# Head 0's attention operands made in place, with q and k loaded a second time with halves exchanged

## What is computed

```python
q_bits = (np.einsum('bhsd,dk->bhsk', q, proj) > 0)      # 6 bits; k_bits in the same way
mask = q_bucket[:, :, :, None] == k_bucket[:, :, None, :]
scores = np.where(mask, scale * q @ k.T, -1e9)
attn = softmax(scores); out = attn @ v
```

## Time and profile before

| | us |
|---|---|
| median of the runs | 743.95 |
| the profiled execution, its device time | 744.51 |
| its span from the first to the last instruction | 742.7 |
| PE busy in the span | 716.0 |
| DVE busy | 427.9 |
| ACT busy | 336.6 |
| POOL busy | 322.8 |

### The profile page before, as it was taken

The page is one execution under the profiler, slowest core; times in us unless marked ns, Lnnn a source line. Parts: engine busy times, 40 slices in busy tenths (PEclk is TensorE's granted clock), DMA queues, the critical chain, the costliest instruction groups (busy, mean ns, idle before and its releaser), DMA issues.

```text
span 742.7 us, 10815 instructions
## 1 busy us (share of the span) xinstructions
PE 716.0 (96%) x3754; PEld 604.6 (81%) x3754; DVE 427.9 (58%) x731; ACT 336.6 (45%) x689; POOL 322.8 (43%) x284
## 2 busy tenths in 40 slices
PE   3999999999998999999999999999999999999998
PEld 2788888888887877788888888888888888888876
DVE  2899999999999777733122121211333556845443
ACT  1899989988987834433210111121223344123101
POOL 3688878878887339855100000020033564221100
PEclk9999999999999999999999999999999999999999
DMA  6464753444332012423000000110011210000002
GB/s 162 117 146 113 176 146 84 99 113 100 88 73 66 1 44 64 135 85 100 0 1 1 0 1 2 41 57 22 1 42 44 85 50 29 1 28 15 15 28 86
DMA packets 39399, 45.76 MB, mean 62 GB/s; under 512 B 15796, under 2 KB 26676, under 8 KB 39348
## 3 DMA queue, kind: packets, MB, share of 16 engines
q1 hardware_dynamic: 36564, 41.65, 20.5%
q0 software_dynamic: 2784, 3.43, 1.8%
HBM read 28.16 MB, written 3.15 MB: 42 GB/s over the span
## 4 chain that ended last, share of the span: by engine, by line
PE 76%; DVE 15%; issue 4%; ACT 2%; DMA 1%; POOL 1%; SPq 0%; ACTq 0%; POOLq 0%; DVEq 0%
PE PS L890 21%; PE PS L892 21%; PE PS L891 21%; DVE negmax L1237 6%; DVE ETL L1247 4%; DVE affine L1240 3%; PE PS L1021 2%; PE PS L981 2%; PE PS L1007 2%; PE PS L1006 2%; PE PS L1022 2%; PE PS L1109 1%; ACT OS L787 1%; PE PS L1036 1%; PE PS L992 1%
## 5 line engine op out<-in xcount | busy, mean ns | idle before, releaser
L1390 DVE SCALAR_TENSOR_TENSOR HL<-PS,HH 128x512 fp32r<-128x512 f32 x48 | 33.1, 691 | 154.7 <-ACT HH L876 154.7
L775 ACT ACTIVATE E<-PS,affine 128x768 f32<-128x768 f32 x96 | 95.2, 992 | 38.8 <-DVE affine L1240 36.1
L876 ACT ACTIVATE HH<-PS 128x512 fp32r<-128x512 f32 x48 | 28.7, 598 | 180.9 <-PE PS L892 180.9
L1237 DVE TENSOR_REDUCE negmax<-PS 128x1 f32<-128x768 f32 x96 | 90.8, 946 | 16.9 <-PE PS L1007 15.8
L1247 DVE TENSOR_TENSOR ETL<-PS,ETH 128x384 fp32r<-128x384 f32 x192 | 97.0, 545 | 2.5 <-ACT ETH L768 2.5
L981 PE MATMUL PS<-ident,E 128*128 128x128 f32 x576 | 81.8, 275 | 2.2 <-DVE ETL L1247 2.1
L768 ACT ACTIVATE ETH<-PS 128x384 fp32r<-128x384 f32 x192 | 82.7, 486 | 0.9 <-PE PS L981 0.8
L1021 PE MATMUL PS<-ETH,VHL 128*128 128x384 f32 x192 | 72.3, 377 | 5.2 <-ACT OS L787 4.7
L890 PE MATMUL PS<-UTH,W 128*128 128x512 f32 x192 | 75.8, 395 | 0.2 <-issue 0.2
L1006 PE MATMUL PS<-TOPH,TOPL 128*128 128x512 f32 x192 | 69.1, 360 | 6.5 <-DMA KM<-MR 6.2
L892 PE MATMUL PS<-UTH,W 128*128 128x512 f32 x192 | 74.8, 390 | 0.0
(11 more groups left out here) (173 smaller groups left out, 1572.2 us busy)
## 6 DMA issues: line engine op xcount, KB each, us to landing
RAW<-in_moe_w_ch_dram SPq DMA_DIRECT2D x32, 256.0 KB, 2.7
QK<-in_qk_dram SPq DMA_DIRECT2D x16, 384.0 KB, 3.8
QM<-TOPH SPq DMA_DIRECT2D x16, 192.0 KB, 2.9
KM<-TOPL SPq DMA_DIRECT2D x16, 192.0 KB, 3.2
VR<-in_v_dram SPq DMA_DIRECT2D x16, 192.0 KB, 2.7
TOPL<-QM SPq DMA_DIRECT2D x16, 192.0 KB, 2.7
TOPH<-TOPH SPq DMA_DIRECT2D x16, 192.0 KB, 3.0
out_dram<-fin SPq DMA_DIRECT2D x12, 256.0 KB, 2.0
```

The source lines that it names most:

```text
L775: nc.scalar.activation(E[:, tile % NE, :], s_bank(tile)[:, 0:S], ACT.Exp, bias=affine[:, t, 1:2], scale=affine[:, t, 0:1], accum_out=esum[ ...
L1237: nc.vector.tensor_reduce(negmax[:, t, 1:2], s_bank(tile)[:, 0:S], AX_X, ALU.max, negate=True).then_inc(s_max, 1)
```

## The change

Head 0 no longer passes through the move DMAs and the mask DMAs.

- The host lays q and k of head 0 into the input a second time, k above q. The load goes to a slice of `E` that is first written by tile 2's exponentials (`turned`). From `QK` and `turned` each of the eight pieces is then made on the partitions where it is used: ACT writes `QM[0:64]` and `TOPL[64:128]`, DVE `TOPL[0:64]`, POOL both halves of `TOPH` and `KM[0:64]`.
- The bits of head 0 come from two matmuls on the fp32 `QK` with the fp32 `proj2`, into a score bank. `proj2` has 44 columns in place of 24: the 12 of q, 20 of zeros, and the 12 of k from column 32 on.
- DVE compares them from PSUM straight into `QM[64:76]` and `KM[64:76]`.
- Two matmuls over a block of zeros stand first on PE.
- ACT's queue issues the three constants; DVE's product of `proj2` waits for two of them.
- Head 1 is split by ACT and DVE in the way of head 0 before, not by POOL. `MB`, `MR` and all bits products have 44 rows in place of 24, for every head.

```diff
@@ sync
             load_qk(0)
-            sp.dma_start(proj2[:], projb).then_inc(s_const, 16)
-            sp.dma_start(sign[:], sign_in).then_inc(s_const, 16)
-            sp.dma_start(gamma[:], gamma_in).then_inc(s_const, 16)
+            sp.dma_start(E[:, NE - 1, :], qk[NH]).then_inc(s_turned, 16)
             load_qk(1)
+            load_v(0)
             sp.dma_start(ident[:], ident_in).then_inc(s_ident, 16)
-            move_away(0)
-            load_v(0)
-            move_in(0)
-            move_mask(0)
             load_qk(2)
             load_v(1)
@@ gpsimd
+            pool.memset(E[:, 0, 0:HC], 0.0).then_inc(s_blank, 1)
...
-            scale_q(1)
+            turned = E[:, NE - 1, :]
...
+            pool.wait_ge(s_qk[0], 16)
+            nc.gpsimd.tensor_copy(TOPH[D:P, 0], QK[D:P, 0]).then_inc(s_first_key, 1)
+            pool.wait_ge(s_turned, 16)
+            nc.gpsimd.tensor_copy(TOPH[0:D, 0], turned[0:D]).then_inc(s_first_key, 1)
+            pool.wait_ge(s_first_key, 2)
+            nc.gpsimd.tensor_tensor(KM[0:D, 0], turned[0:D], TOPH[0:D, 0].bitcast(F32), ALU.subtract).then_inc(s_first_key, 1)
+            pool.wait_ge(s_first_key, 3)
+            split_v(0)
@@ scalar
+            act.dma_start(proj2[:], projb).then_inc(s_const, 16)
+            act.dma_start(sign[:], sign_in).then_inc(s_const, 16)
+            act.dma_start(gamma[:], gamma_in).then_inc(s_gamma, 16)
             act.wait_ge(s_qk[0], 16)
+            nc.scalar.activation(QM[0:D, 0], QK[0:D, 0], ACT.Copy, scale=SCALE).then_inc(s_first_high, 1)
+            act.wait_ge(s_turned, 16)
+            nc.scalar.activation(TOPL[D:P, 0], E[D:P, NE - 1, :], ACT.Copy, scale=SCALE).then_inc(s_first_high, 1)
+            act.wait_ge(s_qk[1], 16)
             act.wait_ge(s_init, 2)
-            nc.scalar.activation(TOPH[:, 0], QK[:, 0], ACT.Copy, scale=qscale[:]).then_inc(s_top, 1)
+            nc.scalar.activation(TOPH[:, 1], QK[:, 1], ACT.Copy, scale=qscale[:]).then_inc(s_top, 1)
@@ tensor
+            blank = E[:, 0, 0:HC]
+            pe.wait_ge(s_blank, 1)
+            for _ in range(2):
+                nc.tensor.matmul(OT, blank[:, 0:P], blank, start=True, stop=True)
+            pe.wait_ge(s_proj, 1)
+            pe.wait_ge(s_qk[0], 16)
+            nc.tensor.matmul(s_bank(1)[0:MW, 0:512], proj2[:], QK[:, 0, 0:512], start=True, stop=True)
+            nc.tensor.matmul(s_bank(1)[0:MW, 512:S], proj2[:], QK[:, 0, 512:S], start=True, stop=True).then_inc(s_first_bits, 1)
...
+                    if tile == 0:
+                        pe.wait_ge(s_first_high, 2)
+                        pe.wait_ge(s_first_key, 3)
+                        pe.wait_ge(s_first_low, 1)
+                        pe.wait_ge(s_first_mask, 2)
@@ vector
-            dve.wait_ge(s_const, 16 * 3)
+            dve.wait_ge(s_const, 16 * 2)
             nc.vector.tensor_tensor(proj2[:], proj2[:], sign[:], ALU.mult).then_inc(s_proj, 1)
...
+            dve.wait_ge(s_first_high, 1)
+            nc.vector.scalar_tensor_tensor(out=TOPL[0:D, 0], in0=QK[0:D, 0], scalar=SCALE, in1=QM[0:D, 0].bitcast(F32),
+                                           op0=ALU.mult, op1=ALU.subtract).then_inc(s_first_low, 1)
+            dve.wait_ge(s_gamma, 16)
+            dve.wait_ge(s_first_bits, 1)
+            nc.vector.tensor_scalar(QM[D:D + NM, 0], s_bank(1)[0:NM, 0:S], gamma[0:NM, 0:1], gamma[0:NM, 1:2], ALU.is_gt,
+                                    ALU.mult).then_inc(s_first_mask, 1)
+            nc.vector.tensor_scalar(KM[D:D + NM, 0], s_bank(1)[KROW:MW, 0:S], gamma[KROW:MW, 0:1], gamma[KROW:MW, 1:2], ALU.is_gt,
+                                    ALU.mult).then_inc(s_first_mask, 1)
```

More of the change, by code:

```diff
@@ L24 @@
 NM = 2 * BITS
+KROW = 32
+MW = KROW + NM
 SCALE = D ** -0.5
@@ L61, in schedule @@
 def schedule():
-    slots = [(None, None, None, [("bits", 0, i) for i in range(2)])]
+    slots = [(None, None, None, [])]
     for n in range(NH * QT):
@@ L108, in program @@
     einv = put("einv", [P, NSTAT])
[L109 to L113, removed]
+    sign = put("sign", [P, MW])
+    proj2 = put("proj2", [P, MW])
+    projH = put("projH", [P, MW], F32R)
+    projL = put("projL", [P, MW], F32R)
+    gamma = put("gamma", [MW, 2])
     stats = put("stats", [P, NT, 6])
@@ L127, in program @@
     region = used[0]
-    MB = put("MB", [2 * NM, S], F32, un_at)
+    MB = put("MB", [MW, S], F32, un_at)
     src_at = tail - 4 * 2 * DM
@@ L158, in program @@
     KM = put("KM", [D + NM, 2, S], F32R)
-    MR = put("MR", [2 * NM, S], F32R)
+    MR = put("MR", [MW, S], F32R)
     VR = put("VR", [P, 2, QT, D])
@@ L550, in split_top @@
                 b, r = h % 2, h % 3
-                pool.wait_ge(s_sq, h)
-                pool.wait_ge(s_top, 2 * h)
+                pool.wait_ge(s_sq, h - 1)
+                pool.wait_ge(s_top, 2 * (h - 1))
                 if h >= 3:
@@ L794, in _ @@
                             act.wait_ge(s_mr, h - 1)
-                        nc.scalar.activation(MB[:, c], ring(unit_no[u])[0:2 * NM, 0:HC], ACT.Copy).then_inc(emptied["bits"], 1)
+                        nc.scalar.activation(MB[:, c], ring(unit_no[u])[0:MW, 0:HC], ACT.Copy).then_inc(emptied["bits"], 1)
                     elif kind == "back":
@@ L984, in unit @@
                     c = slice(i * HC, (i + 1) * HC)
-                    pe.wait_ge(s_top, 2 * (h + 1))
-                    if h == 0 and i == 0:
+                    pe.wait_ge(s_top, 2 * h)
+                    if h == 1 and i == 0:
                         pe.wait_ge(s_proj, 3)
-                    last = product(bank[0:2 * NM, 0:HC], projH[:], TOPH[:, h % 3, c], projL[:], TOPL[:, h % 3, c], True, True)
+                    last = product(bank[0:MW, 0:HC], projH[:], TOPH[:, h % 3, c], projL[:], TOPL[:, h % 3, c], True, True)
                 elif kind == "back":
@@ L1255, in _ @@
                     kind, h, i = u
[L1256 to L1261 removed]
+                    if kind == "s1" and i < 2:
                         half_low(0, i)
@@ L1431, in constants @@
         "ident": np.eye(P, dtype=np.float32),
-        "gamma": np.array([[0, 1]] * BITS + [[-TINY, 1]] * BITS + [[-TINY, -PEN]] * BITS + [[0, -PEN]] * BITS, dtype=np.float32),
-        "sign": np.tile(np.repeat(np.array([[1, -1, -1, 1]], dtype=np.float32), BITS, axis=1), (P, 1)),
+        "gamma": np.array([[0, 1]] * BITS + [[-TINY, 1]] * BITS + [[0, 0]] * (KROW - NM) + [[-TINY, -PEN]] * BITS + [[0, -PEN]] * BITS, dtype=np.float32),
+        "sign": np.tile(np.concatenate([np.repeat([1, -1], BITS), np.zeros(KROW - NM), np.repeat([-1, 1], BITS)]).astype(np.float32), (P, 1)),
         "cs": parts(wave(np.cos, np.arange(S // 2), np.arange(KC), S)),
```

64 lines of the change are left out of this document (35 added, 29 removed).

## The result

The changed kernel takes 742.45 us (median of 17 runs, 741.87 to 743.09), the kernel before beside it 743.93 (17 runs, 743.7 to 744.83). The ratio is 0.998 with a 95% interval of 0.9973 to 0.9988: faster by 1.5 us, where 8 were forecast, and outside the range. The profiled execution took 742.71, its span is 740.4; PE is busy for 720.3 us of it, DVE 433.2, ACT 338.2, POOL 322.4.

What follows compares the result with a forecast made beforehand. Bound by the chain of waits, mostly DMA round trips, before the first score matmul at 14.73 us. An earlier start (6.2) plus clock (1.9) made 8.1 off, forecast 736.0 us, range 734.2 to 740.5.

Steps and rivals of the forecast that it cites:

- T0: Start of the first score matmul: forecast at 8.5 us in place of 14.73, 6.2 earlier, bounds 7.7 to 10.4.
- the clock: PE in the early slots: rises to 2.4 GHz before the first scores and stays, 1.9 us gained, ends 0 and 2.3.
- What bounds the kernel: Start to first scores: mostly three DMA round trips in a row; starting earlier ends the kernel earlier by as much.
- Constants: Loads issued by ACT: second lands at 3.95, with DVE's product 4.2; bounds 3.8 and 5.1 us.
- Order on DVE: DVE before the first scores: head 0's low part runs 4.75 to 5.75, under the bits' matmuls.
- Bits: Head 0's fp32 products on PE: 2.1 us, 4.2 to 6.3; bounds 0.8 and 3.1, or 2.8 by four passes.
- Masks: DVE's two comparisons from PSUM for head 0: 1.07 us each, 6.35 to 8.4, no DMA following.
- cold start: Rival, PE at first scores: still or again at 1.2 GHz, only 6.2 gained, 737.8 us; chance 0.28.
- Reload: Rival, POOL before its subtraction: code library reload of over 1 us delays first scores, middle 739.5 us; chance 0.12.
- POOL paying for rows: Rival, POOL's comparison on 44 rows: grows 2.4 us a head, some 10 us lost, 746; chance 0.04.
- No effect: Rival, after the start: a later wait at an absolute time swallows the gain, 743 to 744 us; chance 0.04.

Runs made afterwards that it cites:

- the delay: Changed kernel with head 0's comparison of q made four times, each waiting for the one before: 745.84 us, ratio 1.0024 to the kernel before.
- the run with wider rows: Kernel before with only the masks' rows widened to 44: 744.79 us, ratio 1.0014 to the kernel before.
- the version of 739.14: Changed kernel with ACT making the signs, projH/projL behind the comparisons, POOL's KM subtraction behind DVE's low part, two more matmuls over zeros between bits and scores: 739.14 us.
- that of 740.51: The version of 739.14 with proj2 on MB's place and no sign tile, so large buffers keep the addresses of the kernel before: 740.51 us, ratio 0.9943.
- the run over zeros: Changed kernel with four matmuls over zeros ahead of the bits and two behind them: 741.90 us, ratio 0.9972 to the kernel before.

## Why the prediction was wrong, point by point

In one line: T0 came 3.35 later than the sum had it, the clock gave nothing of 1.9, and 0.55 was lost behind; 8.1 less these is 2.3, the difference of the two profiled spans (742.7 and 740.4).

**What bounds the kernel: right.** T0 sets the end, and shifts pass nearly one to one (3.53 in, 3.4 out by the delay; 2.85 left at tile 6, 2.62 at tile 95). What it missed is 0.25 us in the heads and 0.3 behind them. The second goes with the addresses; of the first the rows have the larger part, as far as one profile of each version tells, and by a way that stays open. I had costed the rows at nothing and had not thought of addresses.

**Constants: wrong by 1.5 us.** The signs landed at 5.45, not 3.95. Issued at 1.17, as I said, they took 4.28, not `gamma`'s 2.73. My upper bound (5.1) was too low. I chose the row of a load that had gone out behind one big load, where now it leaves on another queue while two big loads are under way. The loads of head 0's q and k and of head 1's took 4.1 in place of 3.3 in the same stretch, and the first constant 3.6. The size of the load is not the reason, by the run with wider rows. Which of the two, the queue or the company, costs the time was not taken apart. It was the first link of the path, so all of it counted.

**Order on DVE: the step that failed by its mechanism.** "4.75 to 5.75, under the bits" for the low part could not be: in program order it stands behind the wait for the signs and three instructions on `proj2`. It came at 8.56. I had costed the product at 0.25 us and the other two at nothing, and POOL held each of them to its own end. The product cost 0.55 more before the bits, and the queue made the comparisons start at 9.54, 0.5 behind the bits in place of 0.05. The rule on the shared port was to be read in the Trainium skill (SBUF — State Buffer, Who interferes with whom), and the case was visible: the change puts POOL's subtraction and DVE's small work at the same time for the first time.

**Bits: a size, 0.7 us.** 2.79 from first start to end, where I took 2.1. The 1.73 between the starts is four times 0.43, as by the rule of the Trainium skill that I cited (FP8 and Floating Point Precision, TensorE Precision Notes; "T0 would be 0.7 later"). It lay inside my bounds; I weighed a row of another operation above the only source on this one. The two matmuls over zeros were dear in the same way, 1.46 each (1.49 to 4.42) and not 0.3, but the bits started only at 6.25.

**Masks: right**, 1.07 each, with 1.10 between their starts and 0.15 to the first matmul, 0.15 more than I had. The sum of the misses: 1.5 + 0.55 + 0.7 + 0.45 + 0.15 = 3.35, and 8.5 became 11.86.

**The clock: nothing of 1.9, the largest single miss.** The step that failed is "PE is busy from 1.5 to 6.3 nearly without a break" and then only about 2 us idle. PE stood still for 1.83 before the bits, which ran at the lower clock, and for 2.81 before T0. Even where the clock was up at the bits, it was down at the scores after 2.63. The rival "cold start" had the outcome; its 0.43 between the first scores is what the trace shows. It had T0 at 8.5 too, so its 737.8 was still 4.7 off. Where the scores did run at the higher clock, the lasting worth was about 0.9, half of my term: tile 4 came 7.87 behind T0 where my chain had 6.9, and tile 6 12.54 where it had 11.3.

**The other rivals: dead.** Reload: POOL's subtraction starts 0.08 us behind the cast (6.14 to 6.22), with the reload between them in program order. The 6 us of the Trainium skill (GPSIMD Engine Reference, Instruction dispatch) are not seen here. POOL paying for rows: 2.93 us for 24 and for 44. No effect: refuted by the delay and by the interval.

**From 2.87 at T0 to 1.5 in the median.** Off go 0.25 and 0.3 by the above: 2.3 in the two profiled spans. Off go 0.6 because the first profile of before was long: 1.7 to 1.8 in median spans (742.1 to 742.2, and 740.4). The time outside the span went from 1.8 to 2.0: 1.5. That last share grew to 2.4 in the version of 739.14 and to 2.8 in that of 740.51. I did not find out why.

## What to carry to other kernels

Before instructions are put on DVE at the start of a path, read what POOL does in the same microseconds: a 0.2 us instruction on SBUF can last until POOL's ends, and what stands behind it in the queue waits too. Walk each engine's queue in program order with its waits, above all the first wait, before saying that something lies "under" other work. A gain in clock has to be protected to the moment where it is used, and behind it: bridge the pauses and look in the profile whether it held, or count nothing for it.

## What the runs showed of the hardware

- DVE's cast of 128x44 took 0.19 us beside an idle POOL and 1.83 or 1.84 beside a subtraction on it, in five kernels. The other way round, POOL's subtraction took 2.50 in place of 1.79 when DVE's instruction had started first.
- An fp32 product of 512 columns is 1.73 us at 1.2 GHz and 0.89 at the higher clock.
- The clock was up before and down after pauses of 1.46, 2.63, 2.64 and 7.44 us, and still up after 0.78 and 1.10. It was up at the bits behind matmuls over zeros as behind ones.
- Where it was down at T0, the first distance of 0.23 or 0.24 came 4.1 to 6.9 us behind T0, and in two profiles of one kernel 2.6 apart.
- The granted clock is no safe sign at the start of a profile. For 12 to 16 us it prints 1.00 in the changed kernel, with starts 0.43 apart; in the run over zeros, with the same distances, it prints 0.50.
- With the buffers moved by 384 bytes a partition, the 490 us from the last tile on were 0.3 us longer, in ten profiles with a move (492.5 to 492.6) against four without (492.2 to 492.3).
- Loads of 22 KB took 3.6 and 4.3 us on a second queue beside two big ones; `gamma` before, less than 1 KB, took 2.73.
